# Second down projection of a three-stage kernel: g becomes the loaded operand, w_out the moving one

## The reference

```python
def reference(x, weight_gen, moe_w_in, moe_w_out, moe2_w_in, moe2_w_out):
    # 1: softmax over 7 taps, then a causal convolution of 7 rows, weights per head and row
    w = softmax(weight_gen, axis=-1)                     # (2, 4096, 8, 7)
    y0 = sum_k w[..., k] * x_padded[:, s + k, head]      # (8192, 192)
    # 2: first feed-forward layer
    h = np.maximum(y0 @ moe_w_in, 0.0)                   # 192 -> 2048
    y1 = h * h @ moe_w_out                               # 2048 -> 192
    # 3: second feed-forward layer
    h = y1 @ moe2_w_in
    g = h * np.cos(h)
    return g @ moe2_w_out                                # (8192, 192), float32
```

## Time and profile before

| | us |
|---|---|
| median of 2 runs | 1189.59 |
| range of these runs | 1189.56 to 1189.62 |
| the profiled execution's own time | 1189.38 |
| its span in the trace | 1187.6 |
| PE busy | 1170.7 (99%) |
| PEld busy | 1101.7 (93%) |
| DVE busy | 962.7 (81%) |
| ACT busy | 808.1 (68%) |
| POOL busy | 366.8 (31%) |

### The profile page before, as it was taken

One profiled execution on the slowest core, in us unless ns is written; L12 is line 12 of the kernel. 1 busy time (PEld: TensorE's weight loads), 2 busy tenths in 40 slices (PEclk: granted clock), 3 DMA queues, 4 the chain that ended last, 5 costly groups with the idle time before them and its releaser, 6 DMA issues.

```text
span 1187.6 us, 25485 instructions
## 1 busy us (share of the span) xinstructions
PE 1170.7 (99%) x9800; PEld 1101.7 (93%) x9800; DVE 962.7 (81%) x1506; ACT 808.1 (68%) x1467; POOL 366.8 (31%) x265
## 2 busy tenths in 40 slices
PE   6999999999999999999999999999999999999998
PEld 5989998899999999999999999999999999999976
DVE  7978888878778787787878878787787878878787
ACT  4877666767666676676667666676666767666675
POOL 3995524070330705115070330705215070000000
PEclk9999999999999999999999999999999999999999
DMA  6512111101111101111001111101111000100000
GB/s 187 143 45 48 35 28 34 17 16 35 25 34 28 35 9 20 34 28 34 15 15 38 24 35 28 34 9 20 34 28 34 14 16 4 25 2 14 1 15 15
DMA packets 113173, 37.32 MB, mean 31 GB/s; under 512 B 101662, under 2 KB 110878, under 8 KB 113052
## 3 DMA queue, kind: packets, MB, share of 16 engines
q1 hardware_dynamic: 111100, 34.87, 14.0%
q10 hardware_dynamic: 1952, 0.80, 0.3%
HBM read 23.84 MB, written 6.29 MB: 25 GB/s over the span
## 4 chain that ended last, share of the span: by engine, by line
PE 91%; DVE 5%; ACT 2%; issue 1%; SPq 0%; DMA 0%; ACTq 0%; DVEq 0%
PE y L598 47%; PE h L598 43%; DVE h L1429 1%; DVE h L1450 1%; DVE g_lo L1462 1%; DVE turns L1435 1%; ACT turns L1138 1%; ACT g_hi L1151 1%; DVE x L1406 0%; DMA xc<-in_x_dram 0%; DVE stat L1285 0%; DVE stat L1276 0%; DVE turns L1315 0%; DVE g_lo L1473 0%; DVE tap L1352 0%
## 5 line engine op out<-in xcount | busy, mean ns | idle before, releaser
L598 PE MATMUL y<-g_hi,wo 64*128 64x512 f32 x3048 | 697.2, 395 | 0.6 <-DVE y_part L1485 0.4
L598 PE MATMUL y<-g_lo,wo 64*128 64x512 f32 x2032 | 524.4, 392 | 0.0
L598 PEld LDWEIGHTS y<-g_hi,wo 64*128 64x128 f32 x3048 | 421.9, 184 | 28.4 <-PE y L598 4.9
L519 POOL TENSOR_TENSOR tap<-xc,gen 128x768 f32<-128x768 f32 x98 | 151.4, 1551 | 582.0 <-DVE xd_lo L1479 566.4
L598 PEld LDWEIGHTS y<-g_lo,wo 64*128 64x128 f32 x2032 | 307.8, 184 | 5.8
L1138 ACT ACTIVATE turns<-turns 128x512 f32<-128x512 f32 x238 | 150.4, 632 | 196.8 <-DVE turns L1435 196.0
L598 PE MATMUL h<-xa_hi,wa_hi 64*128 64x512 f32 x1018 | 273.5, 399 | 0.6 <-DVE g_lo L1473 0.4
L598 PE MATMUL h<-xa_lo,wa_hi 64*128 64x512 f32 x1018 | 269.8, 393 | 0.4 <-DVE g_lo L1320 0.3
L598 PE MATMUL h<-xa_hi,wa_lo 64*128 64x512 f32 x1018 | 268.4, 391 | 0.0
L1450 DVE TENSOR_TENSOR h<-h,turns 128x512 f32<-128x512 f32 x238 | 165.8, 696 | 122.5 <-ACT turns L1138 121.6
L1429 DVE SCALAR_TENSOR_TENSOR h<-h,relu 128x512 f32<-128x512 f32 x249 | 173.2, 696 | 61.4 <-ACT relu L1114 59.2
(11 more groups left out here) (122 smaller groups left out, 1083.8 us busy)
## 6 DMA issues: line engine op xcount, KB each, us to landing
xc<-in_x_dram SPq DMA_DIRECT2D x60, 240.0 KB
out_dram<-arena SPq DMA_DIRECT2D x62, 64.0 KB, 1.9
xt_a<-x_blocks SPq DMA_DIRECT2D x224, 16.0 KB, 1.8
arena<-in_moe_w_out_dram SPq DMA_DIRECT2D x16, 192.0 KB, 3.2
arena<-in_moe_w_in_dram SPq DMA_DIRECT2D x16, 128.0 KB, 2.5
out_dram<-arena SPq DMA_DIRECT2D x62, 32.0 KB, 1.7
xt_d<-x_blocks SPq DMA_DIRECT2D x112, 16.0 KB, 1.8
arena<-in_moe_w_in_dram SPq DMA_DIRECT2D x16, 64.0 KB, 3.0
```

What stands on the lines that cost most here:

```text
L519: pool.tensor_tensor(tap[:, k % 2, :].rearrange("p (r g) -> p r g", g=GROUP), rows[k], wk, ALU.mult).then_inc(pool_step, 1)
L598: return pe.matmul(o, w[rows, :], x[rows, :], start=start, stop=stop)
```

## The change

The second layer's down projection is turned round. For each quarter q of the tile (128 tokens) g is the stationary operand (64 rows by 128 tokens) and w_out the moving one, 192 columns wide, in three products: g high by w high, g high by w low, g low by w high. A step has 4 quarters, 3 products and 2 halves of the array: 24 half products of 192 columns in place of 10 of 512. The result has tokens as rows: quarters 0 and 1 lie in bank 0 of y, 384 columns, quarters 2 and 3 in bank 1. ScalarE copies each bank out (`copy_out`, 128 by 384); the last tile's bank 1 is copied by VectorE. VectorE's add and both transposes go, and so do ScalarE's two copies. SP stores 4 blocks of 32 partitions in place of 8, with 768 bytes in a row of tokens. For the second layer's w_out GpSimd writes one low remainder of 2 by 192 columns in place of two.

The first layer's down projection and both up projections stay as they are. In a slot, `d_first` now has two 512-column products on TOP against six of 192 on BOTTOM, `a_first` three against six, and `downs_last` twelve of 192 on TOP against five of 512 on BOTTOM. The last three steps have 12 products on 128 rows in place of 5 (10 of 256 columns in the last).

```diff
--- before.py
+++ after.py
@@ -135,11 +133,7 @@
         stage_d = arena[:, RING * PIECE:2 * RING * PIECE].rearrange("p (r n) -> p r n", r=RING)
         stage_o = arena[:, 2 * RING * PIECE:STAGE].rearrange("p (r f d) -> p r f d", r=RING, f=PF)
-        y2_d = arena[:, 0:TOK // 2]
-        OUT = TOK // 2
-        out_a = [arena[:, OUT + r * JJ * DM:OUT + r * JJ * DM + TOK] for r in range(2)]
-        out_d = [arena[:, OUT + r * JJ * DM + TOK:OUT + (r + 1) * JJ * DM] for r in range(2)]
+        out = [arena[:, r * QUARTERS * DM:(r + 1) * QUARTERS * DM] for r in range(2)]
         gen = sb("gen", [P, OWN * GEN])
         xc = sb("xc", [P, ROWS * DM])
...
@@ -398,22 +386,11 @@
                 else:
                     rows(q, part * BLOCK // B + 1, (part + 1) * BLOCK // B)
-        def store_a(eng, t, r, blocks):
-            eng.wait_ge(out_a_ready, t + 1)
-            tokens = slice(t * QUARTERS * JJ, (t + 1) * QUARTERS * JJ)
-            for d in blocks:
-                cols = slice(d * BLOCK, (d + 1) * BLOCK)
-                eng.dma_start(out_v[:, tokens, cols],
-                              out_a[r][cols, :].rearrange("n (j c) -> n j c", c=BLOCK)).then_inc(stored[r], 16)
-        def store_d(eng, t, r, blocks):
-            eng.wait_ge(out_d_ready, t + 1)
-            half = QUARTERS * JJ // 2
-            for k in blocks:
-                j0 = t * QUARTERS * JJ + k * BLOCK // DD * half
-                col = DA + k * BLOCK % DD
-                eng.dma_start(out_v[:, j0:j0 + half, col:col + BLOCK],
-                              out_d[r][k * BLOCK:(k + 1) * BLOCK, :].rearrange("n (j c) -> n j c", c=BLOCK)
+        def store(eng, t, r, q0, q1):
+            for j in range(JJ):
+                tokens = slice((t * QUARTERS + q0) * JJ + j, (t * QUARTERS + q1 - 1) * JJ + j + 1, JJ)
+                eng.dma_start(out_v[:, tokens, :],
+                              out[r][j * BLOCK:(j + 1) * BLOCK, q0 * DM:q1 * DM].rearrange("n (q d) -> n q d", d=DM)
                               ).then_inc(stored[r], 16)
         def load_gen(eng, r, quarters=range(QUARTERS)):
...
@@ -647,34 +630,56 @@
                 part_a, part_d = y[:, 0, :], y[:, 1, :]
                 pe.matmul(part_d, w[:, f, DA:2 * P], hi, start=first, stop=False)
                 d_last = pe.matmul(part_d, w[:, f, DA:2 * P], lo, start=False, stop=final)
-                d_last.then_inc(y2_d_done if l else y1_d_done, 1)
+                d_last.then_inc(y1_d_done, 1)
                 pe.matmul(part_a, w[:, f, 0:DA], hi, start=first, stop=False)
                 pe.matmul(part_a, w[:, f, 0:DA], lo, start=False, stop=False)
                 return pe.matmul(part_a, w[:, f, 2 * P:2 * DM], hi, start=False, stop=final)
-            def last_down(k, y, l, f, hi, lo):
-                w = wo[l]
-                for part, cols in parts(k):
-                    part_a, part_d = y[:, 0, cols], y[:, 1, cols]
-                    pe.wait_ge(g2_hi_ready, k + 1 + part)
-                    pe.matmul(part_a, w[:, f, 0:DA], hi[:, cols], start=False, stop=False)
-                    pe.matmul(part_a, w[:, f, 2 * P:2 * DM], hi[:, cols], start=False, stop=False)
-                    pe.matmul(part_d, w[:, f, DA:2 * P], hi[:, cols], start=False, stop=False)
-                if k < STEPS - 1:
-                    pe.wait_ge(g2_ready, k + 1)
-                    pe.matmul(part_d, w[:, f, DA:2 * P], lo, start=False, stop=False).then_inc(y2_d_done, 1)
-                    pe.matmul(part_a, w[:, f, 0:DA], lo, start=False, stop=False).then_inc(down2_done, 1)
+            def down2_product(down, q, j):
+                y, f, hi, lo = down
+                g = (lo if j == 2 else hi)[:, q * P:(q + 1) * P]
+                w = wo[1][:, f, DM:2 * DM] if j == 1 else wo[1][:, f, 0:DM]
+                return y[:, q // 2, q % 2 * DM:(q % 2 + 1) * DM], g, w
+            def down2(down, bank, side, ks, start=False, stop=False):
+                for k in ks:
+                    last = half(*down2_product(down, 2 * bank + k // 3, k % 3), side,
+                                start=start and k == 0 and down[1] == 0,
+                                stop=stop and k == 5 and down[1] == SLOTS - 1)
+                return last
+            def last_down2(down, q, j, stop=False):
+                o, g, w = down2_product(down, q, j)
+                return pe.matmul(o, g, w, start=False, stop=stop)
+            def last_down(k, down):
+                if k == STEPS - 1:
+                    for part in range(2):
+                        pe.wait_ge(g2_hi_ready, k + 1 + part)
+                        for q in range(2 * part, 2 * part + 2):
+                            for j in range(2):
+                                last_down2(down, q, j)
+                    for part in range(2):
+                        pe.wait_ge(g2_ready, k + 1 + part)
+                        last_down2(down, 2 * part, 2)
+                        last_down2(down, 2 * part + 1, 2, stop=True).then_inc(y2_done[part], 1)
                     return
-                (_, cols), (_, cols2) = parts(k)
+                pe.wait_ge(g2_hi_ready, k + 1)
+                for q in range(QUARTERS):
+                    for j in range(2):
+                        last_down2(down, q, j)
                 pe.wait_ge(g2_ready, k + 1)
-                pe.matmul(y[:, 0, cols], w[:, f, 0:DA], lo[:, cols], start=False, stop=False)
-                pe.matmul(y[:, 1, cols], w[:, f, DA:2 * P], lo[:, cols], start=False, stop=False)
-                pe.wait_ge(g2_ready, k + 2)
-                pe.matmul(y[:, 0, cols2], w[:, f, 0:DA], lo[:, cols2], start=False, stop=True).then_inc(down2_done, 1)
-                pe.matmul(y[:, 1, cols2], w[:, f, DA:2 * P], lo[:, cols2], start=False, stop=True).then_inc(y2_d_done, 1)
+                for bank in (1, 0):
+                    last_down2(down, 2 * bank, 2)
+                    last_down2(down, 2 * bank + 1, 2).then_inc(y2_done[bank], 1)
             def down_a(down, side, k, start=False, stop=False):
...
@@ -721,9 +726,11 @@
                 if i == D1 and t > 1:
                     pe.wait_ge(read, t)
-            def y2_free(t, i, read):
+            def y2_free(t, i, m, bank):
                 if i == Y2_AT + 1 and counted(t - 1):
-                    pe.wait_ge(read, t - 1)
+                    pe.wait_ge(out_ready[bank], t - 1)
+                if counted(m - D2):
+                    pe.wait_ge(y2_done[bank], m - D2)
             def downs_of_slot(n, m):
                 k = down_of_slot(n)
...
@@ -970,59 +984,54 @@
                         if m == D2:
                             pe.wait_ge(y1_summed, 1)
                             pe.wait_ge(y1_read, 1)
-                        y2_free(t, i, y2_d_ready)
-                        if counted(m - D2):
-                            pe.wait_ge(y2_d_done, m - D2)
-                        down_d(down2, BOTTOM, 0, start=True)
+                        y2_free(t, i, m, 1)
+                        down2(second, 1, BOTTOM, (0, 1, 2), start=True)
                     down_d(down1, TOP, 1).then_inc(y1_d_left, 1)
                     if two:
-                        down_d(down2, BOTTOM, 1).then_inc(y2_d_left, 1)
-                def d_last():
+                        down2(second, 1, BOTTOM, (3, 4, 5)).then_inc(y2_left[1], 1)
+                def a_first():
+                    y1_free(t, i, y1_read)
+                    pe.wait_ge(down1_done, n - D1)
                     if two:
-                        pe.wait_ge(y2_d_left, m - D2 + 1)
-                        down_d(down2, TOP, 0)
+                        y2_free(t, i, m, 0)
+                    for k in range(3):
+                        last = down_a(down1, TOP, k, start=k == 0)
+                        if k == 2:
+                            last.then_inc(y1_a_left, 1)
+                        if two:
+                            last2 = down2(second, 0, BOTTOM, (2 * k, 2 * k + 1), start=True)
+                            if k == 2:
+                                last2.then_inc(y2_left[0], 1)
+                def downs_last():
                     pe.wait_ge(y1_d_left, downs_in_halves(down_of_slot(n)))
                     down_d(down1, BOTTOM, 0)
                     if two:
-                        down_d(down2, TOP, 1, stop=True).then_inc(y2_d_done, 1)
+                        pe.wait_ge(y2_left[1], m - D2 + 1)
+                        down2(second, 1, TOP, (0, 1))
                     down_d(down1, BOTTOM, 1, stop=True).then_inc(y1_d_done, 1)
-                def a_first():
-                    y1_free(t, i, y1_read)
-                    pe.wait_ge(down1_done, n - D1)
-                    down_a(down1, TOP, 0, start=True)
                     if two:
-                        y2_free(t, i, out_a_ready)
-                        if counted(m - D2):
-                            pe.wait_ge(down2_done, m - D2)
-                        down_a(down2, BOTTOM, 0, start=True)
-                    down_a(down1, TOP, 1)
```

(94 more changed lines are left out.)

116 lines of the change are left out of this document (46 added, 70 removed).

## The result

The changed kernel takes 1219.99 us (median of 2 runs, 1219.96 to 1220.03) against 1189.59 before: a ratio of 1.0255, 95% interval 1.0235 to 1.0276. It is slower, as forecast. The profiled execution took 1220.03 us, its span is 1218.2, 30.6 longer than before.

The account below looks back on a forecast made before the run. PE was taken to bound the kernel, nearly the whole slot being 19 products on each half. Terms 31.4 + 2.3 + 0.1 - 0.8 made +33.0 us on 1189.38, so 1222.4 us, own range 1195 to 1250.

Parts of the forecast that it names:

- Step 1: Second layer's down projection in a slot: 12 products at 0.108 us replace 5 at 0.2325, +0.1335 a step, +31.4 us.
- Step 4: Emptying y2 by two ScalarE copies: counted 0; bounds +7.5 us if the copies don't fit, -2.5 for TensorE's wait.
- Steps 2, 3, 6 and 5: 2: 17 `tail_slot` steps, +2.3 us; 3: last step, +0.1; 6: the end, -0.8; 5: queues, nobody waits.
- Rival A: Products can't start ahead of earlier ones on the array's other half: +87.6, 1277 us; chance 0.13.
- Rival B: Loads hidden, so a 192-column product costs its movement, 0.087 us: a gain, 1158.7 us; chance 0.09.
- Rival C: Narrow products take longer than their load, 0.165 us for 192 columns: 1395 us; chance 0.06.

Follow-up runs that it names:

- experiments with 128 columns: Changed kernel with only the first 128 of 192 columns of w_out moved in each product of the second down projection: 1221.75 us.
- half a load: Changed kernel with 64 of g's 128 columns loaded in slots 1 to 14 of a tile, 192 columns still moved: 1180.16 us.
- one load for two: Changed kernel with high g loaded once to move all 384 columns, 8 loads a step for 12, sums overlapping: 1178.91 us.
- bfloat16: Changed kernel with the second layer's g and w_out in bfloat16, same products: 1165.39 us.

## Why the prediction was right

- **Step 1, the product's cost.** The step was right in kind and small in size: a narrow product is paced by its load. 0.108 was taken, 0.1115 measured; +0.1335 a step was summed and the slot shows +0.167. By itself this would have been +39.2 for 31.4. The experiments with 128 columns and with half a load show the cause from both sides.
- **Step 4, emptying y2.** I counted nothing and kept -2.5. TensorE's wait for the transpose was on the path after all: in the kernel before its removal, with VectorE's other work on y2, gives 2.5 to 3.0. The bound was right and the value taken wrong; that products run on through a load's wait was the failing argument. The other bound, +7.5, didn't come: no new wait of `relu` or PE for the copies.
- **A term that was missing.** The prediction read that the slot of 4.456 is 0.04 longer than its products and gave this no term. It was 0.43 us of stalls in a middle tile, most of it at the tile's start (4.79 for 4.43), and more in the second tile. The longer slot hides it: 8.8 us in all with step 4's, against the 7.8 that step 1 was short. That the two nearly cancel is luck, and the total came out close by it. The three kernels with shorter slots (one load for two, half a load, bfloat16) have such stalls again. How the 8.8 divides between the transpose, `xa_lo` and what the profile calls issue was only partly shown.
- **Steps 2, 3, 6 and 5.** The tail cost 1.1 for 2.4 foreseen, for a reason that no run shows; the end gave 1.0 for 0.8; the queues did nothing visible. The sum was 33.0, the profiles differ by 30.6.
- **Rival A, halves in step.** PE in `d_first` of the changed kernel, where the program has the wide product first and the narrow ones of the other half behind it:
```profile
603.88 0.36 PE L581 MATMUL y<-wo,g_hi 64*128 64x192 f32 x2
603.99 0.39 PE L581 MATMUL y<-g_hi,wo 64*128 64x512 f32 x1
```
  Two narrow ones start from 603.88 on, both before the wide one at 603.99. The pace of 4.584 is far from A's 4.8. The rule of the Trainium skill (TensorE: Matmul & The Clock Gate, Part 3, "What overlaps and what doesn't"), that products start strictly in program order, does not hold between the two halves in this trace. The lead is finite: with the wide products moved behind six narrow ones, 0.07 a slot is lost.
- **Rival B, loads hidden**, was wrong for 128 columns in float32r; with 64 columns (0.087 to 0.089) or in bfloat16 (0.083) it happens. The Trainium skill's formula (TensorE: Matmul & The Clock Gate, "Back-to-back issue gap"), from which the prediction estimated 82.5 ns for 192 columns, is met in bfloat16 alone. The section gives it as the gap of an isolated product and says that in a stream of loads and products both set the spacing, which the prediction left out; the 0.1115 in float32r agrees with that.
- **Rival C, slow narrow products**, fell with both: the distance does not follow the columns below 245, and 0.087 to 0.089 is possible in float32r.

The 0.06 to 0.07 us a slot by which bfloat16 and the half load miss their sums is largely the load of the wide product behind each narrow row, by the starts of loads shown above; no run takes it away. In bfloat16 a change of format lies at both ends of the row, and what that costs by itself was not separated.

## What to carry to other kernels

Price each product at the larger of its moved columns and its own load, here 0.4555 ns a column against 0.1115 us for 128 loaded columns, so a product under some 245 columns pays for its load; fewer moved columns are no gain if they come with more loads. Sharing one load between two products gave 41 us here, though in a kernel whose sums overlap. Count the first wide product behind a row of short ones too: its load has only the short movement to hide under. When the engine that bounds gets slower, look for the once-a-tile stalls that it will hide, and when it gets faster, for those that will come back.

## What the runs showed of the hardware

- A float32r load shows 187 ns for 128 columns and 131 for 64, 56 less; products of 192 columns then stand 0.1115 apart with 128 loaded columns, and 0.087 to 0.089 with 64.
- A load of 128 bfloat16 columns shows 94 ns, half of that, and products of 192 columns stand 0.083 apart; a product of 512 columns then stands 0.215 behind the last one instead of 0.233, although the same columns move.
- The first bfloat16 load behind a float32r product was issued with its own product (601.72), where float32r loads of 512-column products went 0.23 ahead. Within a row of bfloat16 products the loads do go ahead (load at 603.37, its product at 603.45).
- Products of one half of the array can start ahead of waiting ones of the other half that stand before them in the program. Two did so in the changed kernel, and a wide one that stood behind six narrow ones started with the fourth (602.82).
